# A float32 attention and mixture kernel: the first weight set is asked for with the first pair of heads, and VectorE in place of GpSimd makes the first two sets' low parts

## What is computed

```python
# q, k, v: (8, 8, 576, 64), heads of batch entries
kv  = einsum('bhsd,bhse->bhde', k, v)
out = einsum('bhsd,bhde->bhse', q, kv)
out = out / sqrt(mean(out * out, axis=-1) + 1e-6) * g_norm
x = out.transpose(0, 2, 1, 3).reshape(4608, 512)
x = (sigmoid(x @ w_gate) * (x @ w_val)) @ w_out      # d_ff 1536
h = x @ w_in                                         # d_ff 2048
g = where(h >= 1, h, where(h <= -1, 0, (h + 1)**2 / 4))
return g @ w_out2
```

## Time and profile before

| | us |
|---|---|
| median of 3 runs | 1652.26 |
| lowest and highest | 1650.11, 1653.1 |
| the profiled execution | 1651.67 |
| its span from first to last instruction | 1649.8 |
| TensorE busy in the span | 1636.5 (99%) |
| VectorE busy | 1217.3 (74%) |
| ScalarE busy | 887.9 (54%) |
| GpSimd busy | 213.1 (13%) |

### The profile page before, as it was taken

How to read it: one execution, slowest core, us unless ns; L and a number is a source line. 1 busy time by engine, 2 the same in 40 slices (tenths; PEclk the granted TensorE clock), 3 DMA queues, 4 the chain that set the end, 5 groups by cost and what they waited for, 6 DMA issues and landing times. The chain is left out here.

```text
span 1649.8 us, 31817 instructions
## 1 busy us (share of the span) xinstructions
PE 1636.5 (99%) x12458; PEld 1616.1 (98%) x12458; DVE 1217.3 (74%) x1733; ACT 887.9 (54%) x1616; POOL 213.1 (13%) x277
## 2 busy tenths in 40 slices
PE   8999999999999999999999999999999999999999
PEld 6899999999999999999999999999999999999999
DVE  5777777778776776877878877777777686666664
ACT  5666666655555554544445555555555444444443
POOL 6300002025222321100102500000001200000000
PEclk9999999999999999999999999999999999999999
DMA  8544444244667678645634433323438964444450
GB/s 272 182 132 144 145 137 153 101 134 134 198 223 255 231 243 287 237 167 183 198 120 164 155 131 130 139 110 127 169 144 275 342 191 128 128 129 129 132 137 27
DMA packets 232966, 278.91 MB, mean 169 GB/s; under 512 B 33136, under 2 KB 177008, under 8 KB 232816
## 3 DMA queue, kind: packets, MB, share of 16 engines
q1 hardware_dynamic: 220752, 233.35, 43.0%
q0 software_dynamic: 12064, 43.52, 8.1%
HBM read 156.76 MB, written 120.06 MB: 168 GB/s over the span
## 5 line engine op out<-in xcount | busy, mean ns | idle before, releaser
L1665 PE MATMUL x<-t_hi,v_lo 128*128 128x288 f32 x1664 | 495.1, 298 | 2.9 <-DVE t_lo L1168 1.9
L1666 PE MATMUL x<-t_lo,v_hi 128*128 128x288 f32 x1664 | 491.1, 295 | 0.0
L1667 PE MATMUL x<-t_hi,v_hi 128*128 128x288 f32 x1664 | 490.0, 294 | 0.0
L1665 PEld LDWEIGHTS x<-t_hi,v_lo 128*128 128x128 f32 x1664 | 312.2, 188 | 6.3 <-ACT kept L960 1.7
L1667 PEld LDWEIGHTS x<-t_hi,v_hi 128*128 128x128 f32 x1664 | 313.5, 188 | 0.0
L1666 PEld LDWEIGHTS x<-t_lo,v_hi 128*128 128x128 f32 x1664 | 312.8, 188 | 0.2
L1665 PE MATMUL y<-t_hi,v_lo 128*128 128x288 f32 x832 | 247.0, 297 | 0.5 <-DVE c_tile L1171 0.3
L1666 PE MATMUL y<-t_lo,v_hi 128*128 128x288 f32 x832 | 245.6, 295 | 0.0
L1667 PE MATMUL y<-t_hi,v_hi 128*128 128x288 f32 x832 | 244.9, 294 | 0.0
L1665 PE MATMUL x<-v_hi,t_lo 128*128 128x256 f32 x576 | 163.2, 283 | 0.0
L1666 PE MATMUL x<-v_lo,t_hi 128*128 128x256 f32 x576 | 163.0, 283 | 0.0
(11 more groups left out here) (202 smaller groups left out, 3546.3 us busy)
## 6 DMA issues: line engine op xcount, KB each, us to landing
g_scratch<-c_tile SPq DMA_DIRECT2D x128, 288.0 KB, 2.4
gq<-g_scratch SPq DMA_DIRECT2D x64, 512.0 KB, 6.3
h_scratch<-gate SPq DMA_DIRECT2D x192, 144.0 KB, 2.0
hq<-h_scratch SPq DMA_DIRECT2D x32, 864.0 KB, 5.3
stage<-w_in POOLq DMA_DIRECT2D x68, 256.0 KB, 3.8
fold_hi<-v_hi SPq DMA_DIRECT2D x14, 896.0 KB, 6.1
fold_lo<-v_lo SPq DMA_DIRECT2D x14, 896.0 KB, 7.6
kv_ring<-kv_in SPq DMA_DIRECT2D x24, 512.0 KB, 4.5
```

Source lines behind the costliest of these rows:

```text
L1665: nc.tensor.matmul(dst, s_lo, m_hi, start=start, stop=False, skip_group_check=True)
L1666: nc.tensor.matmul(dst, s_hi, m_lo, start=False, stop=False, skip_group_check=True)
L1667: return nc.tensor.matmul(dst, s_hi, m_hi, start=False, stop=stop, skip_group_check=True)
```

## The change

It has five parts. GpSimd asks for task 0 right after its first constant instead of after all constants and after pair 0's landing. Task 1 is asked for after pair 2's landing instead of pair 3's. The low parts of tasks 0 and 1 go from GpSimd to VectorE: one instruction of 128x1792 in place of seven of 128x256. VectorE sums task 0 ahead of its copies of pairs 0 and 1, and ScalarE makes its high part ahead of the first squares. Around the second round some instructions trade places: the second inverse's low part comes ahead of item 1's, one scaling on ScalarE comes ahead of the root, and item 4's sum goes behind the low parts of items 2 and 3.

```diff
 GpSimd
+            make(nc.gpsimd.memset(kv_raw[:], 0.0))
+            load_task(0)
...
-            pool.wait_ge(first_kv_loaded[0], 32)
-            load_task(0)
-            pool.wait_ge(first_kv_loaded[3], 32)
+            pool.wait_ge(first_kv_loaded[2], 32)
             load_task(1)
@@
-                if task == 0:
-                    split_first(0)
-                elif FOLD2_TASK <= task < C_TASK:
+                if FOLD2_TASK <= task < C_TASK:
                     sum_right(task)
-                else:
+                elif task:
+                    if task == 1:
+                        pool.wait_ge(v_hi_done, 1)
                     sum_left(task)
@@
-                if task == 1:
-                    split_first(1)
 ScalarE
+            split_weights(0)
             for c in range(2):
                 square_heads(0, c)
                 scale_heads(0, c)
             root(0)
-            split_weights(0)
@@
-            root(1)
             scale_heads(0, 2)
+            root(1)
             scale_heads(0, 3)
 VectorE
+            sum_weights(0)
             copy_first(0)
             copy_first(1)
-            sum_weights(0)
+            split_weights(0)
             invert(0)
@@
             invert(1)
-            split_item(0, 1)
             split_inverse(1)
+            split_item(0, 1)
@@
             sum_item(0, 2)
-            sum_item(0, 4)
             split_item(0, 2)
             split_item(0, 3)
@@
+                if k == 0:
+                    sum_item(0, 4)
                 if s == 0 and b < A_BLOCKS:
                     split_item(b, 4)
+                if k == 0:
+                    split_weights(1)
```

More of the change, by code:

```diff
@@ L639, in make @@
                 pool.wait_ge(const_ready, made)
[L641 to L659, removed]
             def load_pair(task, weights, a, b, crossed):
@@ L727, in load_d @@
                 load_factor(fold2_dram, QUAD_D[ORDER_D[x // 2]], 4 * (x % 2), d_pieces(x), d_loaded[x])
[L729 to L736, removed]
-            pool.wait_ge(first_kv_loaded[0], 32)
-            load_task(0)
-            pool.wait_ge(first_kv_loaded[3], 32)
+            heads = [slice(j * D, (j + 1) * D) for j in range(P // D)]
+            make(nc.gpsimd.memset(kv_raw[:], 0.0))
+            load_task(0)
+            make(nc.gpsimd.memset(head_cols[:], 0.0))
+            make(nc.gpsimd.memset(head_r[:].bitcast(f32), 0.0))
+            for j, rows in enumerate(heads):
+                make(nc.gpsimd.memset(head_cols[rows, 16 + j:49 + j:32], 1.0 / D))
+                make(nc.gpsimd.memset(head_r[rows, 16 + j:49 + j:32].bitcast(f32), 1.0 / D))
+            make(nc.gpsimd.memset(eps_col[:], EPS))
+            ones = flat(kept[:])[:, 0:2 * H * D]
+            make(nc.gpsimd.memset(ones, 0.0))
+            make(nc.gpsimd.memset(inv_pair[:].bitcast(f32), 0.0))
+            blocks = ones.rearrange("r (h d) -> r h d", h=2 * H)
+            for first_row in (0, 32):
+                make(nc.gpsimd.affine_select(out=blocks, in_=blocks, compare_op=ALU.not_equal, fill=1.0, base=-first_row,
+                                             pattern=[[-1, 2 * H], [0, D]], channel_multiplier=1))
+            pool.wait_ge(const_ready, CONSTANTS)
+            nc.gpsimd.memset(half_col[:], 0.5).then_inc(const_ready, 1)
+            assert made == CONSTANTS
+            pool.wait_ge(first_kv_loaded[2], 32)
             load_task(1)
@@ L941, in _ @@
             split_item(0, 0)
+            scale_heads(0, 2)
             root(1)
-            scale_heads(0, 2)
             scale_heads(0, 3)
@@ L1189, in split_weights @@
                 dve.wait_ge(v_hi_done, task + 1)
-                if task == 2:
-                    dve.wait_ge(v_ready, 2)
                 for base, first, count in chunk_pieces(task):
@@ L1401, in _ @@
             invert(1)
+            split_inverse(1)
             split_item(0, 1)
-            split_inverse(1)
             normalize_part(0, 2, 0)
```

## The result

The changed kernel took 1656.46 us (median of 9 runs, 1654.29 to 1658.17) against 1653.46 us for the kernel before beside it (9 runs, 1650.11 to 1655.44): a ratio of 1.0019, 95% interval 1.001 to 1.0028. It is slower by 3.0 us; forecast was a gain of 1.2 us, and 1656.46 lies above the range. The profiled execution took 1658.03 us, with a span of 1656.2.

A forecast was written before the change was run, and what follows sets the result against it. TensorE, nearly always busy in the main loop, was taken as the bound, so step 1's start decides. A gain of 2.07 less a later start of 0.9 gave 1.2 us: 1650.9 us forecast, range 1648.6 to 1653.6.

The forecast's parts named there:

- What bounds the kernel: TensorE is almost never idle in the main loop, so time won or lost before step 1 reaches the end almost whole.
- Parts 1 to 4: From the second inverse to step 1, with low parts on VectorE: step 1 starts at 36.45 instead of 38.52, gaining 2.07 us.
- Part 5 (a): At the start, GpSimd's constants end later and ScalarE makes set 0's high part before the squares: second mean +0.35 us.
- (c): At the start, VectorE waits for and sums set 0 before copying pair 0, then makes its low part: mostly hidden.
- Part 5 (b): Set 0's early 512 KB, worth 1.4 us at 371 GB/s, delay pair 0's end by 0.9 us and the mean by 0.8.
- R1: The slow clock stays or moves, so step 1 starts near 37.7 and nothing changes: 1651.8 us; chance 20%.
- R2: Set 0 holds VectorE at the head of its queue: start +2.5 to +4.5 us, time 1652.5 to 1654.7; chance 18%.
- its point of 8.2: Set 0 landing after 8.2 us was to mean a start later than 2.07 us, so a slower kernel.
- R3: The start costs nothing, the same bytes moving in another order: gain 2.07 us or more, 1649.6 to 1650; chance 17%.
- R4: Set 0 is asked for early but lands no sooner; its chance is counted within R2.
- the start's bound of 3: The upper bound, in us, on the later start, which was forecast at 0.9 with a lower bound of 0.
- the clock's 1.7: Within R2, a TensorE idle time at the start may drop its clock for a stretch, costing 1.7 us.

The follow-up runs named there:

- e10: e2 without the new order around the second round, so only the low parts moved to VectorE remain; 1650.06 us, ratio 0.9974.
- e9: The kernel before with only the new order around the second round, low parts still on GpSimd; 1655.48 us, ratio 1.001.
- e1: The kernel before with only GpSimd's early ask for set 0 added; 1655.98 us, ratio 1.002.
- e4: The kernel before with only half of set 0 (256 of 512 KB) asked for early by GpSimd; 1655.09 us, one run.
- e8: The kernel before with set 0 asked for by SyncE in its own queue, behind the rest and query 0; 1654.77 us, one run.
- e11: The kernel before with an extra 16 KB load by GpSimd at the early place; 1653.97 us, one run.
- e3: The changed kernel with 18 more matmuls into an unused bank inside the wait for the key-value rest; 1655.21 us, ratio 1.001.
- e5: The changed kernel a second time, with nothing altered; 1655.6 us, one run.
- e6: The changed kernel with SyncE asking for the key-value rest first and the small norm factors last; 1656.53 us, ratio 1.0019.
- e2: The changed kernel with the start of the kernel before, so set 0 is asked for late; 1651.99 us, ratio 0.9999.
- e7: e2 with SyncE asking for the key-value rest first and the small norm factors last; 1651.17 us, ratio 0.9986.
- e12: e2 once more, timed in a second set of rounds; 1651.7 us, ratio 0.9989.

## Why the prediction was wrong, by its own steps

**What bounds the kernel** held: what step 1 lost (3.24) came out in the medians (3.0).

**Parts 1 to 4** held: 2.07 us were forecast and 2.31 measured. Taken from the mean's end, product 6 starts 2.06 sooner (1.94 forecast), the wait before the spread is 0.62, the new one before product 7 is 1.20 where 1.5 stood, and ScalarE ends it, as said. The low parts of set 1 (2.02 us from 39.68) let step 1 start without a wait. The cause was named for the right row: GpSimd's seven subtractions beside VectorE; e10 and e9 show that without and with them. The gain doesn't rest on the clock that fell in the one profile of before: from the mean's end to step 1 the old second half took 22.8 to 23.6 us in five profiles (before, e1, e4, e8, e11), only one of them with a fall, and the new one 21.3 to 21.4 in four (the change, e3, e5, e6). What I did not see is that the reorder inside this sum earns nothing of its own.

**Part 5 (a)** was priced at 0.35 and cost nothing: ScalarE's copy began at 8.07 (7.7 forecast), its high part at 11.05, and then it stood idle for 1.89 us before the square of heads 0. It was hidden altogether, behind a pair 0 that was 3.85 us late. **(c)** was right: hidden in the first profile, 0.5 us in e5.

**Part 5 (b) is the step that failed.** It priced set 0 by bytes at the steady 371 GB/s, 1.4 us, and took +0.9 on the end of pair 0. It came to +3.85 there. Three things were wrong in it. The rate was that of a later stretch: in 4 to 8 us both kernels move 236 to 253 GB/s, and I had a stretch of that time at hand in the same trace. At 253 GB/s the same bytes are worth 2.1 us. Then the loads of SyncE were not merely preceded by set 0: its queue fell to 0.49 MB in 4 us while GpSimd's took 0.45, so nearly half of the bytes moved were ones that TensorE did not need for another 20 us (product 1 of step 0 began at 28.91). And the sentence on the Trainium skill (DMA: Bandwidth & Descriptors, Queues, rings and completion order), that each DMA engine takes turns between its queues, stood there with an effect on the first pair (which was not touched: its two DMAs took 3.1 us to landing, 3.0 before) and was given no price for the rest. The two queues' rows agree with it, and so does e8, where one queue makes the same bytes cost 1.1 us. By my estimate from it the rest should be about the bytes of GpSimd later, 2.1 us, and it was 3.6; and half of those bytes, in e4, should have cost half, and cost as much as all in e1. What fills the remaining 1.5 us stays open. The five profiles with an early ask by GpSimd landed the rest in about the order of their flow in 8 to 12 us (11.5 and 10.9 at 267 and 266 GB/s, 9.7 at 319, 9.1 and 9.0 at 338 and 339), against 378 in before. In 4 to 8 us the flow doesn't stand in that order (193, 236, 208, 250 and 196), and 8 to 12 us lies in part behind the landing, so this is no explanation either.

**The clock** was the second half of the miss, 2.0 us by e3. I looked for a fall after the wait ahead of product 6 (R1) and at the start only within R2, as an effect of VectorE being held. It came within TensorE's wait of 4.31 us for a load. R1's fall between 31 and 38 did not come: from 15.98 to 43 us all is at 1.00.

**The rivals.** R2 gave the right sign and was short: 1654.7 at most (and its lower end, +0.4, is 1652.7, not 1652.5), and its mechanism was wrong. Set 0 landed at 9.4, after its point of 8.2, but VectorE finished the sums before pair 0 was done, as its timeline shows:

```profile
9.47 0.42 DVE L1160 TENSOR_TENSOR stage<-stage 128x256 f32<-128x256 f32 x1 [8.33 <-DMA stage<-w_in]
9.81 1.21 DVE L1163 TENSOR_TENSOR stage<-stage 128x256 f32<-128x256 f32 x3
11.78 0.47 DVE L1188 COPY kv_raw<-z 64x64 f32<-64x64 f32 x2 [0.76 <-PE z L1675]
```

The price came through the rest of the key-value rows. R3 and R4 are out. The sum that would have held is: load +3.55, clock +2.0, second half -2.31, together +3.24. The range failed because the start's bound of 3 and the clock's 1.7 were not carried to its end: 3 + 1.7 - 2.07 is +2.6, or 1654.9 from the median then known. Another 1.2 us is no effect of the change: the median of before rose by that between the first 3 runs and the 9.

## What to carry to other kernels

A transfer that is asked for early is not free because the DMA engines look unfilled: price it by the rate of the stretch in which it will run, and ask whose bytes it runs beside. Here, asked for by a second queue from the first microseconds on, it took a share from the loads on which the next product waited; in the queue that carried those loads, behind them and asked for 2.4 us later, it cost only what stood after it (e8, one profile). And where a new wait of some us lands on TensorE, add to the bound what the clock may take after it.

## What the runs showed of the chip that I had not expected

- **Waits and the clock, at the start.** The grant fell to 0.5 after or in waits of 4.31 (after), 3.05 (e5), 2.83 (e4), 1.97 (e6), 1.91 (e1) and 1.36 us (e10), and stayed low for 3.4 us (e1, e10) to 10.2 us (e6); it did not fall where the wait was 1.12 and less (e2, e7, e8, e9, e11, e12), nor in e3, where the 18 matmuls left 1.30 us of waiting. The length of one wait doesn't decide it: at product 6 a wait of 1.55 us was followed by a fall in before, one of 1.56 us in e11 was not, and neither was the 2.11 us ahead of product 7 in e9.
- **The start of the DMA engines.** In 4 to 8 us they were busy for 0.82 to 0.96 of the time and moved 236 to 253 GB/s in the two kernels (193 in e3, 301 in e6), in 12 to 23 us 371 GB/s in before.
- **Two engines on SBUF.** The low part of an item on VectorE took 0.75 to 0.76 us with GpSimd idle (the change, e10) and 1.14 to 1.29 us beside its subtractions (before, e9, e11), a sum of that size 1.31; the reciprocal took 1.93 to 1.95 us in every profile, beside GpSimd's sums (23.92 to 27.2 in before) or not.
